# New instruction orders on every queue, and the channel layer's residual added on VectorE from DRAM instead of through TensorE transposes

## The reference, cut to what matters

```python
# q, k, v: (4 batches, 8 heads, 576 tokens, 64)
scores = q @ k.T / 8, masked to 0 <= i - j < 64      # sliding window of 64
x = softmax(scores) @ v                              # -> (4, 576, 512)
h = relu(x @ w_in); u, v = h[..., :512], h[..., 512:]
v = (v - mean(v)) / sqrt(var(v) + 1e-6)              # over the 512 channels
y = (u * (w_spatial @ v + b_spatial[:, None])) @ w_out
z = y + (relu(y.T @ w_tok1) @ w_tok2).T              # token layer, residual over tokens
out = z + relu(z @ w_ch1) @ w_ch2                    # channel layer, 512 -> 1536 -> 512
```

## Time and profile before

| | |
|---|---|
| median of 3 runs | 713.12 us (712.9 to 713.96) |
| the profiled execution | 713.94 us |
| span of its instructions | 712.1 us |
| TensorE matmul busy | 686.2 us, 96% |
| VectorE, ScalarE, GpSimd busy | 308.9, 241.9, 153.1 us |
| mean granted TensorE clock | 0.993 |

### The profile page before, as it was taken

One profiled execution on the slowest core, in us unless ns is written; L12 is line 12 of the kernel. 1 busy time (PEld: TensorE's weight loads), 2 busy tenths in 40 slices (PEclk: granted clock), 3 DMA queues, 4 the chain that ended last, 5 costly groups with the idle time before them and its releaser, 6 DMA issues.

```text
span 712.1 us, 11482 instructions
## 1 busy us (share of the span) xinstructions
PE 686.2 (96%) x4205; PEld 632.7 (89%) x4205; DVE 308.9 (43%) x859; ACT 241.9 (34%) x660; POOL 153.1 (22%) x237
## 2 busy tenths in 40 slices
PE   5799988999999999999999999999999999999998
PEld 5588888889998899999999999998999998999996
DVE  4965896665946668465472321121121121121110
ACT  5555345523546235462337311221211221211211
POOL 3732325521226212252146700000000000000000
PEclk9989999999999999999999999999999999999999
DMA  8857014250052400103423200200200200200101
GB/s 166 237 141 123 1 35 83 52 134 1 1 97 44 128 2 1 31 4 120 153 92 109 92 20 1 89 0 1 88 0 0 88 0 0 90 1 0 45 1 44
DMA packets 99073, 41.21 MB, mean 58 GB/s; under 512 B 85968, under 2 KB 89616, under 8 KB 99024
## 3 DMA queue, kind: packets, MB, share of 16 engines
q1 hardware_dynamic: 99024, 40.56, 22.0%
HBM read 31.11 MB, written 9.44 MB: 57 GB/s over the span
## 4 chain that ended last, share of the span: by engine, by line
PE 88%; DVE 5%; issue 2%; ACT 2%; SPq 1%; POOL 1%; DMA 0%; DVEq 0%; POOLq 0%; ACTq 0%
PE ps L1086 66%; PE ps L1182 10%; PE ps L1126 4%; PE ps L1151 4%; PE ps L1136 2%; SPq L478 1%; PE ps L1327 1%; PE ps L1245 1%; DVE att L888 1%; DVE arena L923 1%; ACT att L699 1%; DVE att L908 1%; PE ps L1105 1%; DVE att L871 0%; DVE den L897 0%
## 5 line engine op out<-in xcount | busy, mean ns | idle before, releaser
L1086 PE MATMUL ps<-arena 128*128 128x288 f32 (+3 forms) x2064 | 360.2, 326 | 2.4 <-DVE arena L912 1.7
L1086 PEld LDWEIGHTS ps<-arena 128*128 128x128 f32 (+1 forms) x2064 | 324.4, 187 | 20.7 <-issue 3.0
L1086 PE MATMUL ps<-arena,att_r 128*128 128x512 f32 x648 | 161.1, 393 | 0.0
L1019 DVE SCALAR_TENSOR_TENSOR att_r<-ps,att_r 128x384 fp32r<-128x384 f32 x72 | 40.1, 558 | 250.3 <-ACT att_r L785 250.3
L1086 PEld LDWEIGHTS ps<-arena,att_r 128*128 128x128 f32 x648 | 120.6, 188 | 22.0
L785 ACT ACTIVATE att_r<-ps 128x384 fp32r<-128x384 f32 x72 | 35.4, 492 | 252.1 <-PE ps L1086 252.1
L1182 PE MATMUL ps<-arena 128*128 128x288 f32 (+1 forms) x560 | 95.6, 321 | 0.1
L1182 PEld LDWEIGHTS ps<-arena 128*128 128x128 f32 x560 | 80.6, 190 | 4.1 <-DVE arena L999 1.0
L617 POOL TENSOR_SCALAR att<-att,rinv 128x128 f32<-128x128 f32 x144 | 56.1, 408 | 94.8 <-DVE rinv L899 94.6
L699 ACT ACTIVATE att<-att,nmax 128x128 f32<-128x128 f32 x144 | 56.0, 391 | 37.7 <-DVE nmax L888 37.7
L1151 PE MATMUL ps<-att 128*128 128x128 f32 x288 | 39.6, 285 | 6.3 <-DVE att L908 5.8
(11 more groups left out here) (78 smaller groups left out, 479.1 us busy)
## 6 DMA issues: line engine op xcount, KB each, us to landing
u_scratch<-uy SPq DMA_DIRECT2D x16, 288.0 KB, 3.0
out_dram<-att SPq DMA_DIRECT2D x18, 256.0 KB, 2.1
att<-in_v_dram SPq DMA_DIRECT2D x16, 256.0 KB, 3.8
att<-in_q_dram SPq DMA_DIRECT2D x48, 72.0 KB, 2.6
att<-in_k_dram SPq DMA_DIRECT2D x48, 72.0 KB, 2.6
att<-in_moe_w_ch_dram SPq DMA_DIRECT2D x8, 384.0 KB, 5.6
att<-in_moe_w_ch_dram SPq DMA_DIRECT2D x6, 512.0 KB, 3.7
xT<-u_scratch SPq DMA_DIRECT2D x3, 768.0 KB, 4.8
```

Of the source, the lines that this page charges most:

```text
L1019: dve.scalar_tensor_tensor(out=h3[:, j % RING, 1, :], in0=ps[:, 6 + j % 2, 0:CK], scalar=0.0, in1=h3[:, j % RING, 0, :].bitcast(F32), op0= ...
L1086: ins = pe.matmul(dst, w[a], x[c], start=first and n == 0, stop=last and n == 2, skip_group_check=True)
```

## The change

All of the orders are new strings. The names in them are the same but for two new kinds. The excerpts below are those that the prediction uses.

The residual of stage 2 takes another way. After te of a batch, DVE transposes each 128-channel block of uy in 32x32 blocks (`ut`, four per batch, 128x576 each) into turn_at: three areas in the room of t1, and for the fourth block the gate buffer. SP stores each with four DMAs of 32 partitions in 128-byte pieces (`sr`) to a second DRAM scratch with tokens as rows. In stage 2 SP loads three tiles of 128 tokens of it per chunk into `rest`. DVE, not ACT, empties the output banks and adds `rest` in the same instruction. The 12 transposes of each chunk are gone from TensorE.

There are new waits. ACT's uu waits for ut of the batch before; ACT's ah waits for the stores of three turned blocks, and DVE's first sa for the fourth, since they share the memory. At the start of stage 2 SP waits for all 64 sr DMAs and for the last channel weight before it loads `rest` and chunk 1. The load of the next chunk no longer waits for the transposes but for the low part of the present chunk.

```diff
 PROLOGUE_PE
-Q0 K0 S0 S1 Q1 K1 S2 Q2 K2 T0 S3 T1 V0 S4 V1 T2 S5 T3 v0 + V2 V3 T4 T5 V4 V5 v1 Q3 K3 + Z4 S6 S7 v2 S8 +
+Q0 K0 Q1 S0 K1 S1 S2 K2 S3 Q2 T0 V0 S4 T1 S5 V1 T2 T3 V2 V3 T4 v0 T5 V4 V5 Q3 + K3 v1 + Z4 S6 S7 v2 S8
...
 PROLOGUE_DVE
-... m4 r3 hv0 hv1 hv2 hv3 m5 lv0 xl0 lv2 r4 r5 c2 c3 hu0 hu1 hu2 hu3 vs0 vo3 c4 c5 xl1 vn0
+... hv0 hv1 lv0 m4 c1 r3 hv2 r4 m5 c2 c3 xl0 r5 vo2 c4 hv3 c5 lv2 xl1 vo3 hu0 hu1 hu2 ke3 vs0 xl2 m6 vn0
...
 FIRST_PE
-g00 + g10 + g20 + g30 + g01 + g11 S0 + g21 S1 + g31 S2 + y00 +
+g00 + g10 + S0 S1 g20 + g30 + g01 + g11 + g21 + g31 S2 T0 S3 + y00 +
+... S8 T6 V5 v0 + V6 T7 b00 ... b31 v1 V7 T8 + V8 v2 + v3 + v4 + u00 + ... u31 +
...
 FIRST_DVE
-sa00 sm00 sa10 gl00 ho0 sm10 ho1 sa20 gl10 ho2 sm20 ho3 sa30 gl20 ha0 sm30 ha1 qt0 sa01
+qt0 ho0 ha0 qt1 sa00 qt2 sa10 sm00 m0 sm10 gl00 ho1 ho2 sa20 gl10 sm20 sa30 ha1 sm30 gl20 ho3 r0 sa01 m1
...
 EPILOGUE_PE
-... a3 a4 H0 b00 b10 b20 b30 b01 b11 b21 b31 H1
+... a3 a4 H0 H1 b00 b10 b20 b30 b01 b11 b21 b31
 EPILOGUE_DVE
-... al0 al1 H0 te00 te10 te20 te30 te01 te11 te21 te31 H1
+... al0 al1 te00 H0 te10 te20 te30 te01 te11 te21 te31 ut0 H1 ut1 ut2 ut3
 ALL_SP
+... lk20 lv14 st00 st01 lv20 st02 sr00 lq20 lv21 st03 sr01 sr02 sr03 lv22 ...
+... st30 wb410 wb411 st31 wb412 sr30 wb413 sr31 sr32 st32 st33 sr33
...
+                if kind == "sr":
+                    sp.wait_ge(u2_turned, KD * b + x + 1)
+                    for i in range(4):
+                        sp.dma_start(rows_dram[b * S:(b + 1) * S, x * P + 32 * i:x * P + 32 * i + 32].rearrange("(j p) n -> p j n", p=32),
+                                     turn_at[x][32 * i:32 * i + 32, :].rearrange("p (j n) -> p j n", n=32)).then_inc(rows_stored[x], 16)
...
             for m in range(KD):
                 sp.wait_ge(u2_stored[m], 16 * B)
+                sp.wait_ge(rows_stored[m], 64 * B)
+            sp.wait_ge(w_ready, NB)
+            for t in range(TT):
+                sp.dma_start(rest[:, 0, t, :], rows_dram[t * P:(t + 1) * P, :]).then_inc(rest_in[0][t], 16)
...
-                    sp.wait_ge(o_open, c + 1)
+                    sp.wait_ge(ub_lo, c + 1)
                     sp.dma_start(u2f[1 - par], u2_dram[:, :, bass.ds((c + 1) * CK, CK)]).then_inc(u2_in[1 - par], 16)
+                    for t in range(TT):
+                        sp.dma_start(rest[:, 1 - par, t, :], rows_dram[bass.ds((c + 1) * CK + t * P, P), :]) \
+                            .then_inc(rest_in[1 - par][t], 16)
...
+                    act.wait_ge(u2_turned, KD * (b - 1) + m + 1)
...
+                if b > 0 and x == 0:
+                    dve.wait_ge(rows_stored[KD - 1], 64 * b)
                 dve.wait_ge(*unit_full(("g", b, x)))
...
+            def turn_residual(b, m):
+
+                if b > 0:
+                    dve.wait_ge(rows_stored[m], 64 * b)
+                dve.wait_ge(acc_dve, ACC_DVE["te", b, 10 * m + 1])
+                dve.transpose(turn_at[m], uy3[:, m, :]).then_inc(u2_turned, 1)
...
-                    act.activation(osb[:, i, :], ps[:, OBANKS[par][t], :], ACT.Copy).then_inc(o_copied, 1)
...
+                dve.wait_ge(w_ready, NB)
+                for t in range(TT):
+                    i = OSB[par][t]
+                    dve.wait_ge(rest_in[par][t], 16 * it + 16)
+                    dve.wait_ge(o_stored[i], 16 * stores_before(it, par, t))
+                    dve.wait_ge(o_full, TT * c + t + 1)
+                    dve.tensor_tensor(osb[:, i, :], ps[:, OBANKS[par][t], :], rest[:, par, t, :], ALU.add).then_inc(o_copied, 1)
...
-                for t in range(TT):
-                    for m in range(KD):
-                        ins = pe.matmul(o[t][:, m * P:(m + 1) * P], u2f[par][:, m, t * P:(t + 1) * P], ident[:, :],
-                                        is_transpose=True, start=m == 0, stop=False, skip_group_check=True)
-                ins.then_inc(o_open, 1)
...
                         ins = product(o[t], [h3[:, j % RING, s, t * P:(t + 1) * P] for s in range(2)],
-                                      [ch2_s[:, j, s, :] for s in range(2)], False, j == KC - 1)
+                                      [ch2_s[:, j, s, :] for s in range(2)], j == 0, j == KC - 1)
```

More of the change, by code:

```diff
@@ L71, in bass_attention_gmlp_mixer_kernel @@
[L71 removed]
+        "g00 + g10 + g20 + g30 + g01 + g11 + g21 + g31 + y00 + y10 + y20 + y30 + y01 + y11 + t0 t1 y21 + y31 + a0 "
+        "t2 a1 t3 t4 a2 a3 a4 H0 H1 b00 b10 b20 b30 b01 b11 b21 b31").split()
     PROLOGUE_ACT = (
[L73 to L74 removed]
+        "qe0 qe1 e0 e1 qe2 e2 e3 o0 e4 o1 xh0 e5 o2 o3 xh1 o4 o5 qe3 xh2 vr0 vr1 ze4 e6 vh0 e7 e8 wh0 vr2 o6 uu00 "
@@ L86, in bass_attention_gmlp_mixer_kernel @@
+        "th1 yy21 wb7 yy31 uf0 th2 wb8 th3 th4 ah0 ah1 wb9 H0 H1 wb10 wb11 wb12 wb13").split()
     PROLOGUE_DVE = (
-        "ke0 m0 m1 ke1 vo1 r0 m2 r1 ke2 vo2 c0 m3 r2 c1 m4 r3 hv0 hv1 hv2 hv3 m5 lv0 xl0 lv2 r4 r5 c2 c3 hu0 hu1 "
-        "hu2 hu3 vs0 vo3 c4 c5 xl1 vn0 xl2 ke3 vl0 vs1 m6 m7 vo4 vn1 m8 r6 r7 vs2 r8 vl1 c6 c7 vn2 vl2 c8 xl3 xl4 "
-        "vs3 wl0 vn3 vs4 wl1 vl3 vn4 wl2 wl3 vl4 kt0 wl4 wl5 kt1").split()
+        "ke0 m0 ke1 m1 r0 m2 ke2 vo1 r1 c0 m3 r2 hv0 hv1 lv0 m4 c1 r3 hv2 r4 m5 c2 c3 xl0 r5 vo2 c4 hv3 c5 lv2 "
@@ L90, in bass_attention_gmlp_mixer_kernel @@
+        "xl1 vo3 hu0 hu1 hu2 ke3 vs0 xl2 m6 vn0 hu3 m7 r6 m8 vs1 r7 vl0 r8 wl0 c6 vs2 c7 vo4 vn1 c8 kt0 xl3 vl1 "
+        "wl1 vn2 xl4 wl2 kt1 wl3 vl2 wl4 vs3 vs4 vn3 wl5 vn4 vl3 vl4").split()
     FIRST_DVE = (
[4 rows of a table removed]
-        "vl3 vn4 vl4").split()
[4 rows of a table added]
+        "vs4 ut3 vn4 vl3 vl4 kt1").split()
     LOOP_DVE = (
[3 rows of a table removed]
-        "te11 te21 kt1 te31 vs0 vn0 vs1 vl0 vn1 vs2 vl1 vn2 vs3 vl2 vn3 vs4 vl3 vn4 vl4").split()
[3 rows of a table added]
+        "vn0 te01 te11 te21 vn1 vl0 vl1 te31 ut0 vs2 ut1 vn2 vl2 vs3 vn3 vs4 ut2 ut3 vl3 vn4 vl4 kt1").split()
@@ L101, in bass_attention_gmlp_mixer_kernel @@
     EPILOGUE_DVE = (
-        "sa00 sm00 gl00 sa10 sm10 sa20 gl10 sm20 sa30 gl20 sm30 sa01 gl30 sm01 sa11 gl01 sm11 sa21 gl11 sm21 sa31 "
-        "gl21 sm31 gl31 tl0 tl1 tl2 tl3 tl4 al0 al1 H0 te00 te10 te20 te30 te01 te11 te21 te31 H1").split()
+        "sa00 sm00 gl00 sa10 sa20 sm10 gl10 sa30 sm20 sm30 gl20 sa01 sm01 gl30 gl01 sa11 sm11 sa21 gl11 sa31 sm21 "
+        "sm31 gl21 gl31 tl0 tl1 tl2 tl3 tl4 al0 al1 te00 H0 te10 te20 te30 te01 te11 te21 te31 ut0 H1 ut1 ut2 ut3").split()
     PROLOGUE_POOL = (
-        "n0 n1 n2 n3 lv1 lv3 n4 n5 lu0 lu1 lu2 lu3 rs0 rs1 n6 n7 n8 rs2 rs3 rs4").split()
+        "n0 n1 lv1 n2 n3 n4 n5 lv3 lu0 lu1 rs0 lu2 lu3 n6 rs1 n7 n8 rs2 rs3 rs4").split()
@@ L294, in bass_attention_gmlp_mixer_kernel @@
         tp = ps[:, 6:8, :]
+        turn_at = [early[:, START["t1"] - START["w_out"] + i * S:START["t1"] - START["w_out"] + (i + 1) * S] for i in range(3)]
+        turn_at.append(gate[:, :, :].rearrange("p s n -> p (s n)"))
+        assert 3 * S <= SIZES["t1"] and 2 * HALF == S
+        rows_dram = nc.dram_tensor("u2_rows", (B * S, DM), F32, kind="Internal").ap()
         u2_dram = nc.dram_tensor("u2_scratch", (P, KD, B * S), F32, kind="Internal").ap()
@@ L769, in token_high @@
                         act.wait_ge(*piece_lo("b", i))
+                elif c == 0:
+                    for m in range(3):
+                        act.wait_ge(rows_stored[m], 64 * b)
                 act.wait_ge(*unit_full(("acc_a", b, c)))
@@ L1065, in _, with chunk @@
                     piece_low(kind[1:], b, x)
-            def chunk(c, par, last):
+            def chunk(c, it, par, last):
                 for j in range(2, KC):
```

59 lines of the change are left out of this document (30 added, 29 removed), and 24 rows, old and new, of tables (ALL_SP, FIRST_DVE, LOOP_DVE, LOOP_PE).

## The result

| | before | changed |
|---|---|---|
| median | 713.52 us (4 runs) | 691.19 us (4 runs, 691.04 to 693.31) |
| the profiled execution | 713.94 us | 691.28 us |
| span | 712.1 us | 689.4 us |
| TensorE matmul busy | 686.2 us | 670.6 us |
| mean granted clock | 0.993 | 0.997 |

The account below looks back on a forecast made before the run. TensorE was taken as the bound, with 88% of what ended last. 713.94 - 7.9 (transposes) - 6 (prologue) - 5 (segment 2) + 0.5 (start of stage 2) + 0.1 (last add) = 695.6, stated as 695 us, range 687 to 706.

Parts of the forecast that it names:

- The transposes, 7.9: Stage 2: removing six chunks' transposes of 1.31 us each from TensorE gains 7.86 us, all on the path.
- VectorE's turns, 0: Stage 1: four transposes a batch, 2.7 us, cost nothing; 11 us if all were on the path.
- SP's queue, 0 but close: Stage 1: sixteen more issues a batch at 0.60 us cost nothing, with 1 to 2.7 us to spare in segment 2.
- The start of stage 2, +0.5: Chunk 0: TensorE waits 0.6 us, taken as 0.5, for chunk 1's z, loaded only after all turned blocks are stored.
- C: Rival: stage 1 as forecast, but stage 2's start stalls 3 to 5 us from slow stores or load; 698 to 700, chance 0.11.
- Two of the prediction's signs: Stage 2: ScalarE's split starts 21 to 23 us into chunk 0; a chunk above 50.3 us would prove the forecast wrong.
- The prologue, -6 (2 to 9): Prologue: moving c4, c5 ahead removes 3.00 us of idle time and 3 us of half clock; gain 6, bounds 2 and 9.
- Segment 2, -5 (0 to 8): Segment 2: S0, S1 behind g10 and qt0 first remove the wait at 91.00 us and its clock; gain 5 us.
- Segments 3 and 4, 0: Segments 3 and 4: together 1.2 us of idle time, so no change; bounds a gain of 1 and a loss of 3.
- The epilogue, at nothing: Epilogue: the hidden pair moved ahead of b costs and brings nothing.
- Rival B: Rival: the new orders only move the waits and stage 1 gains 3 us or less; 703, up to 706, chance 0.22.
- D: Rival: dear issues on SP's queue, 1.5 us instead of 0.60, make it 5 us slower, 718; chance 0.07.

Follow-up runs that it names:

- residual_only: The kernel before with its old orders and only the residual's new path (turns and stores) put in; 706.05 us.
- weights_first: The changed kernel with the last four channel-weight loads moved ahead of st30 on SP's queue; 687.71 us.
- late_c4_c5: The changed kernel with the copies c4 and c5 moved behind lv2, xl1, vo3 and hu0 to hu2 in VectorE's prologue list; 702.09 us.
- old_second: The changed kernel with segment 2's old lists on TensorE, ScalarE, VectorE and GpSimd, turns added, new SP list kept; 719.42 us.
- early_load: The kernel of `weights_first` with chunk 1's z loaded ahead of the last eight sr; 686.69 us, repeated at 685.82 us.
- late_q: The changed kernel with q's transposes and S0, S1 back in their old places in segment 2, e0 behind gh30; 694.04 us.
- orders_only: The kernel before with all the new orders but without ut and sr, TensorE's transposes kept; 696.95 us.

## Why the forecast came out as it did

**The transposes, 7.9.** Right: `residual_only` gave 7.7, on its own. The add takes 682 ns (0.689 forecast), and no matmul waits for it; only the last stores do, as the forecast had it:

```profile
L1111 DVE TENSOR_TENSOR att<-ps,att 128x512 f32<-128x512 f32 x18 | 11.4, 682 | 3.8 <-PE ps L1123 3.8
```

**VectorE's turns, 0.** Right. A turn takes 768 ns where I said half of 1.368, and the segments that have them have no idle time on TensorE.

```profile
L1039 DVE STREAM_TRANSPOSE early<-uy 128x576 f32<-128x576 f32 x12 | 9.1, 768 | 0.3 <-issue 0.3
```

**SP's queue, 0 but close.** Right, and close: twice the issues cost 20.7 us, 5.6 of it in segments 2 to 4. Eight sr took 4.90 us, and the slack was used where I had counted it, as ScalarE's uu30 did wait for st03:

```profile
148.04 4.90 SPq L557 DMA_DIRECT2D u_rows<-early  x8
```

```profile
151.14 0.41 ACT L771 ACTIVATE uy<-ps 128x288 f32<-128x288 f32 x1 [0.45 <-DMA u_scratch<-uy]
```

**The start of stage 2, +0.5.** The chain that I counted was right and not the one that mattered. With the weights out of the way it gives 0.88 us at hidden group 8 for a forecast of 0.6 (`weights_first`). In the changed kernel an earlier wait of 4.28 + 1.4 us hides it. The step that failed is the sentence "A new wait ends last here: chunk 1's z": I followed the new DMAs to their readers and counted the weight load between them only as part of 1.3 us of issues, but never asked who waits for that weight. So the size of C came, and a little more, by another mechanism than C's. Of C's own mechanism there is a trace: the sixteen sr landed in a median of 3.6 us in that full stretch (2.2 to 6.0) where I had 3.0, and chunk 1's load in 5.6 for 4.7. With the weights ahead the same sr landed in 2.1, which speaks for the load on the DMA engines and against the shape of the pieces. Two of the prediction's signs fell with this step: ScalarE's split of chunk 1 started at about 25.5 us of chunk 0 instead of 21 to 23 (22 in `weights_first`), and chunk 0 took some 55.9 us, where the prediction called itself wrong above 50.3.

**The prologue, -6 (2 to 9).** Right in kind, low in size: 9.2, just over the bound. The step that failed in size is "5.4 us out from in front of V4 and V5 ... 6 us": I took only the visible idle time and its clock, and called the rest latency of the first blocks. TensorE's idle time fell from 14.2 to 10.05 us and its busy time from 62.75 to 57.72, with the granted clock up from 0.96 to 1.00; `late_c4_c5` shows that none of it comes without the early c4 and c5.

**Segment 2, -5 (0 to 8).** It gave 10.3, out of the bounds, and its step fell: "S0 and S1 stand behind g10, with qt0 first in VectorE's list, so that the wait ... go". Undoing that costs 1.5 us in the segment. And I priced one wait, of the segment's 7.3 us of idle time. The next one, for probabilities, is in the kernel before:

```profile
112.04 2.02 PE L1151 MATMUL ps<-att 128*128 128x128 f32 x16 [2.31 <-DVE att L908]
```

`old_second` has both again, 3.64 and 2.27 us, so they belong to the segment's old lists on the four engines. I also wrote that gates and GpSimd's subtractions meet in the new order too; the first gates do not. Which of the moves carries how much I did not test.

**Segments 3 and 4, 0.** They gave 1.6 and 0.75, together more than the bound of 1, and both are now at 89.01.

**The epilogue, at nothing.** It cost 1.1, the gates beside wb0, which I had not looked at.

The sum: 9.2 - 6 = 3.2 and 10.3 - 5 = 5.3 and 2.4 in the loops more than I forecast, less 5.2 more lost at the start of stage 2, 1.1 in the epilogue and the rest below 1: 695.6 became 691.3. The forecast stood by luck in part: it was 10.9 us too low in what the orders of stage 1 bring and 6.3 too low in what stage 2's start and the epilogue lose, and the two partly cancelled. Rival B fell (stage 1 gained 22 us to the last g00). So did D: it wanted 1.25 us an issue, and eight sr in segment 2 took 0.61 each; only four, at the start of stage 2, came near, 1.19 each.

The same prologue lists put g00 at 67.77 to 70.19 us in different profiled executions, and the traces show two reasons. In `early_load`, the latest, the granted clock was 0.78 from 24 to 36 us, where the others had 1.00. In `late_q` (69.17) VectorE waited for w_in, as it did for 1.65 us in `orders_only` (69.54) and 1.52 in `weights_first` (68.73), and for nothing there in the changed kernel:

```profile
35.24 2.19 DVE L942 CAST arena<-early 128x512 fp32r<-128x512 f32 x3 [2.47 <-DMA early<-in_moe_w_in_dram]
```

Why the clock fell in one execution only, and the load came later in some, is open.

## What to carry to other kernels

When a step moves in an in-order queue, list every waiter of everything behind it, old work too: here the dearest new wait was for a weight load that did not change, only its neighbours did. The lists of one stretch are one object, SP's among them: swapping some of them cost more than the change had gained there. Keep GpSimd's two-input subtractions off the moments when TensorE waits for VectorE's two-input steps. And where a chain names a releaser, compare the count that the code waits for: here it named a subtraction that nothing waited for.
